# Where the streamed operands of TensorE's matmuls lie in SBUF against their weights

## The reference, cut to what matters

```python
mask = q_bucket[:, :, :, None] == k_bucket[:, :, None, :]
scores = scale * np.matmul(q, k.transpose(0, 1, 3, 2))
scores = np.where(mask, scores, -1000000000.0)
attn = np.exp(scores - max); attn = attn / (sum + 1e-09)
x = attn @ v                                   # (2, 768, 512)
```

```python
x = (sigmoid(causal_conv5(x)) * (x @ w_val)) @ w_out
xk = mu_k * x + (1 - mu_k) * x_prev            # x_prev: the token before
xr = mu_r * x + (1 - mu_r) * x_prev
k = np.maximum(xk @ w_k, 0.0)                  # 512 -> 1024
out = sigmoid(xr @ w_r) * (k * k @ w_v)        # 1024 -> 512
```

## Time and profile before

| | us |
|---|---|
| median of 3 runs | 484.28 (484.23 to 484.29) |
| the profiled execution | 484.03 |
| its span | 482.2 |
| TensorE matmul rows busy | 472.4 (98%) |
| TensorE weight-load rows busy | 401.4 (83%) |
| VectorE, ScalarE, GpSimd busy | 345.7, 279.4, 259.8 |
| TensorE on the chain that ended last | 79% of the span |
| scores L688, 384 matmuls | 92.1 busy, 361 ns each |
| dense matmuls L735 and L743, streamed 256 columns | 277 to 283 ns each |

### The profile page before, as it was taken

One profiled execution on the slowest core, in us unless ns is written; L12 is line 12 of the kernel. 1 busy time (PEld: TensorE's weight loads), 2 busy tenths in 40 slices (PEclk: granted clock), 3 DMA queues, 4 the chain that ended last, 5 costly groups with the idle time before them and its releaser, 6 DMA issues.

```text
span 482.2 us, 9492 instructions
## 1 busy us (share of the span) xinstructions
PE 472.4 (98%) x3541; PEld 401.4 (83%) x3541; DVE 345.7 (72%) x607; ACT 279.4 (58%) x597; POOL 259.8 (54%) x258
## 2 busy tenths in 40 slices
PE   7899999999999999999999999999999999999997
PEld 6766767676676776777779999999999999999997
DVE  5887897988888888887747977876678579326211
ACT  5977878878787987876745541442443353344230
POOL 5795647374472745652197673575455457346140
PEclk9999999999999999999999999999999999999999
DMA  6210310304021030200220001001000000100101
GB/s 231 67 55 18 113 41 5 135 17 137 16 68 72 17 136 18 71 19 18 88 87 1 3 1 44 1 1 46 2 2 32 13 2 1 45 1 2 44 1 44
DMA packets 10557, 20.69 MB, mean 43 GB/s; under 512 B 1680, under 2 KB 6928, under 8 KB 10512
## 3 DMA queue, kind: packets, MB, share of 16 engines
q1 hardware_dynamic: 10224, 19.94, 12.4%
q10 hardware_dynamic: 288, 0.15, 0.1%
HBM read 16.94 MB, written 3.15 MB: 42 GB/s over the span
## 4 chain that ended last, share of the span: by engine, by line
PE 79%; DVE 9%; issue 5%; ACT 3%; POOL 2%; DMA 1%; SPq 0%; DVEq 0%; POOLq 0%; ACTq 0%
PE ps L735 29%; PE ps L723 14%; PE ps L743 12%; PE ps L699 10%; PE ps L688 10%; ACT probs L500 2%; PE ps L709 2%; DVE gate L923 1%; DVE tmp_b L1014 1%; DVE negmax L880 1%; DVE pt L887 1%; PE ps L671 1%; DVE x L913 1%; PE ps L662 1%; DMA raw_k<-kT 1%
## 5 line engine op out<-in xcount | busy, mean ns | idle before, releaser
L880 DVE TENSOR_REDUCE negmax<-ps 128x1 f32<-128x768 f32 x96 | 91.7, 956 | 23.6 <-PE ps L688 22.9
L688 PE MATMUL ps<-k,q 128*128 128x384 f32 x384 | 92.1, 361 | 3.4 <-ACT probs L500 2.8
L500 ACT ACTIVATE probs<-ps,negmax 128x768 f32<-128x768 f32 x96 | 86.6, 902 | 10.2 <-DVE negmax L880 9.9
L699 PE MATMUL ps<-ident,probs 128*128 128x128 f32 x576 | 82.3, 275 | 1.2
L699 PEld LDWEIGHTS ps<-ident,probs 128*128 128x128 f32 x576 | 66.8, 140 | 11.9 <-DVE pt L887 4.7
L688 PEld LDWEIGHTS ps<-k,q 128*128 128x128 f32 x384 | 62.7, 189 | 15.3 <-ACT probs L500 10.6
L723 PE MATMUL ps<-pt,vals 128*64 128x384 f32 x384 | 68.8, 494 | 0.0
L450 POOL TENSOR_TENSOR h_lo<-tmp_b,h_hi 128x256 fp32r<-128x256 f32 x48 | 38.9, 816 | 45.3 <-ACT h_hi L602 45.3
L508 ACT ACTIVATE pt<-ps 128x384 f32<-128x384 f32 x96 | 47.0, 489 | 18.7 <-PE ps L699 15.0
L887 DVE COPY pt<-ps 128x384 f32<-128x384 f32 x96 | 52.1, 542 | 2.8 <-PE ps L699 2.8
L735 PE MATMUL ps<-xk_hi,w_hi 128*128 128x256 f32 x192 | 53.7, 280 | 0.0
(11 more groups left out here) (86 smaller groups left out, 1105.4 us busy)
## 6 DMA issues: line engine op xcount, KB each, us to landing
w_raw<-w SPq DMA_DIRECT2D x8, 640.0 KB, 6.4
raw_q<-qT SPq DMA_DIRECT2D x8, 384.0 KB, 5.2
raw_k<-kT SPq DMA_DIRECT2D x8, 384.0 KB, 3.2
vals<-v SPq DMA_DIRECT2D x16, 192.0 KB, 2.4
out<-w_raw SPq DMA_DIRECT2D x24, 128.0 KB, 1.7
w_raw<-w SPq DMA_DIRECT2D x4, 512.0 KB, 3.3
codes_b<-codes ACTq DMA_DIRECT2D x1, 128.0 KB, 4.2
proj_bd<-proj ACTq DMA_DIRECT2D x1, 16.0 KB, 3.3
```

The source lines that it names most:

```text
L500: act.activation(probs[par][:, :], score[par], ACT.Exp, bias=negmax[:, t:t + 1], accum_out=sums[:, t, 0:1]).then_inc(exp_done, 1)
L688: last = pe.matmul(ps[:, 2 * par + half, 0:HALF], qq[h][:, q], kk[h][:, half * HALF:(half + 1) * HALF], start=first, stop=not first)
L699: last = pe.transpose(tbank[u][:, k * P:(k + 1) * P], probs[g % 2][:, kt * P:(kt + 1) * P], ident[:, :])
L880: dve.tensor_reduce(negmax[:, t:t + 1], score[g % 2], AX.XY, ALU.max, negate=True).then_inc(max_done, 1)
```

## The change

Only declarations change, so only addresses. In the attention a set is declared as `q1`, `q2`, a filler of 64 bytes (`KEYS_BEHIND`), `k1`, `k2`, and after the three sets a filler of 320 bytes rounds the fillers up to 512. In the dense part the filler before `x_hi` becomes 288 bytes, the one before `y_hi` goes, the one before `h_hi` becomes 64, the one before `xk_hi` 448, and the one before `xr_hi` goes. Program order, waits and transfers are as before.

```diff
+KEYS_BEHIND = (64, 64, 64)
...
-        def apart(name, size):
+        def apart(name, size, stack=ctx):
 
-            sb(f"apart_{name}", [P, size // 4])
+            sb(f"apart_{name}", [P, size // 4], F32, stack)
...
             q1[s] = sb(f"q1_{s}", [P, SEQ], F32R, att)
+            q2[s] = sb(f"q2_{s}", [P, SEQ], F32R, att)
+            apart(f"k_{s}", KEYS_BEHIND[s], att)
             k1[s] = sb(f"k1_{s}", [P, SEQ], F32R, att)
-            q2[s] = sb(f"q2_{s}", [P, SEQ], F32R, att)
             k2[s] = sb(f"k2_{s}", [P, SEQ], F32R, att)
+        apart("sets", -sum(KEYS_BEHIND) % 512, att)
...
-        apart("x", 256)
+        apart("x", 288)
         x_hi, x_lo = sb("x_hi", [P, DT, GQ], F32R), sb("x_lo", [P, DT, GQ], F32R)
-        apart("y", 448)
         y_hi, y_lo = sb("y_hi", [P, DT, GQ], F32R), sb("y_lo", [P, DT, GQ], F32R)
...
-        apart("h", 288)
+        apart("h", 64)
         h_hi, h_lo = sb("h_hi", [P, FT, GQ], F32R), sb("h_lo", [P, FT, GQ], F32R)
-        apart("xk", 32)
+        apart("xk", 448)
         xk_hi, xk_lo = sb("xk_hi", [P, DT, GQ], F32R), sb("xk_lo", [P, DT, GQ], F32R)
-        apart("xr", 288)
         xr_hi, xr_lo = sb("xr_hi", [P, DT, GQ], F32R), sb("xr_lo", [P, DT, GQ], F32R)
```

## The result

The changed kernel takes 486.00 us (median of 7 runs, 485.86 to 486.33), the kernel before 484.28 us: 1.0033 times as long, interval 1.0023 to 1.0044. It is slower, by 1.7 us, where 6.0 us less was forecast. Its profiled execution took 485.88 us.

A forecast was written before the change was run, and what follows sets the result against it. The prediction took TensorE's start-to-start matmul time as the bound in the dense part; savings of 4.4 + 0.5 + 1.1 = 6.0 us gave 478.3 us. Its range was 475.0 to 482.3 us.

The forecast's parts named there:

- What bounds the kernel: TensorE's stream of load and matmul pairs in the dense part; layout can move the time from start to start.
- Step A: From 317.2 us on: all x, y, xk and h stages fall to 113.3 ns a matmul, 4.4 us less.
- Step B: From 235 to 317.2 us: 2.2 us by the same arithmetic, mostly lost in waits, so 0.5 us less.
- Step C: Attention scores: 8.3 ns less a matmul with keys 64 behind queries; a third counts, 1.1 us less.
- slow lock: Rival: after the wait at 317.21 us the dense stream stays at 117.9 ns a matmul; 485.8 us, chance 0.09.
- stages near 118 ns: Sign that the forecast is wrong: dense stages at 118 ns a matmul, pointing to the slow lock.
- scores still at 175 ns: Sign that the forecast is wrong: attention score matmuls still start 175 ns apart, instead of 166 to 168.

The follow-up runs named there:

- xk_288: The changed kernel with xk_hi and xk_lo moved back to 288 behind their weights, all else at 64; 482.38 us.
- w0_64: The changed kernel with w2 at the place of w1 modulo 512, dense operands still 64 behind their weights; ten executions from 479.6 to 485.8 us, ratio 0.9988.
- keys_only: The kernel before with only the attention's new sets, dense fillers as before; 483.78 us, ratio 0.9994 (0.9985 to 1.0003).
- kick: The changed kernel, no address changed, with one extra small matmul ahead of the y stage of chunks 2, 3, 4 and 5; 485.77 us.
- w0_192: The changed kernel with w2 at the place of w1 modulo 512 and all dense operands at 192; ten executions from 478.9 to 485.8 us, ratio 0.9968.
- w0_192_kick: w0_192 with one extra matmul of 128 columns ahead of the y stage of chunk 2; median 479.72 us, ratio 0.9936.
- x_32: The changed kernel with x alone at 32 behind its weights; twelve executions, eight of them at 485.6 to 486.1 us, ratio 1.0012.

## Why the prediction was wrong

**What bounds the kernel** held: the distance from one dense matmul's start to the next is the time of the second half, and all of the 1.8 us came from it.

**Step A failed, the forecast -4.4 us, measured +1.8 us.** It took 113.3 ns for a property of the offset 64, because five of six xr stages had it. Those five were no five witnesses: each was entered the same way, from an xk at 288 in its changing rhythm (starts 113 to 120 ns apart, 116.7 on average), in one execution. The sixth, entered from a wait by way of a steady xk, was the other state of the same layout, and the changed kernel's profile has that state in 27 of its 30 dense stages. An xk in the changing rhythm is no guarantee either: in xk_288 the one at 299.93 us was followed by a long xr. The arithmetic behind it was sound: w0_64 shows 1392 matmuls at 113.3 ns in its short executions and a time of 479.6 to 480.0 us.

**Step B** was tested only in part. The y and x from 249 us on were short, and nearly all of their gain went into the wait behind them: x's last start to xk's first grew from 0.25 to 0.65 us, and xk began 0.07 us earlier, where 0.1 us was forecast. The stages from there to 317 us were long, and the wait there shrank instead of growing: y began 0.05 us later, not 0.5 us earlier.

**Step C was mis-sized.** The excess of the scores was to fall by 8.3 ns a matmul. In the changed kernel they are still (105.80 - 105.45) / 2 = 175 ns apart in the tile that the earlier trace rows shows for before, and the attention's 213 us hold the same 1354 matmuls.

```profile
105.45 0.33 PE L689 MATMUL ps<-k,q 128*128 128x384 f32 x1
...
105.63 0.33 PE L689 MATMUL ps<-k,q 128*128 128x384 f32 x1
...
105.80 0.34 PE L689 MATMUL ps<-k,q 128*128 128x384 f32 x1
```

keys_only bounds the effect by its interval to 0.7 us less, where 1.1 us was forecast. The excess taken from streams of 256 columns did not carry over to streams of 384; why, no run shows.

**The rival "slow lock"** named the outcome and its size: 485.8 us, measured 486.0, with +0.88 us for xr, +0.62 for h and +0.46 for xk; from the stage starts they are 4 x 48 x 4.5 = 0.86, 480 x 1.2 = 0.58 and 384 x 1.0 = 0.38 us. That its total fits so well is partly luck: it holds 0.5 us back from the scores, which did not come, and its stages add up to 2.0 us where 1.8 came. It got a chance of 0.09, by counting stages. Its account of where the rhythm is decided was half right. The wait at 317 us can give either rhythm (w0_64 is the same program with either), but in the changed kernel it would hardly matter if the boundary from h to x ends a short one there as it did in xk_288 and kick, at the same addresses. The forecast looked at the offset of each stage and not at the one stream and load that meet across two stages.

Of the signs that the prediction named, stages near 118 ns and scores still at 175 ns came true.

**What stays open.** What makes 64 and 192 good and 0 and 96 bad, what puts a stage after a wait into one rhythm or the other, and whether any entry can force the short one. Only steps of 32 bytes were tried, several in one execution each. No short execution of w0_192, w0_192_kick or x_32 was profiled.

## What to carry to other kernels

A distance between starts seen in one stage may be one of two stable states of the same layout; before a layout is changed for it, look how each stage with that distance was entered, and treat stages that follow each other in one execution as one observation. When streams and weights are laid out against each other, the boundary between two stages counts as well: from h to x the good state lasted only in the kernels with a filler that put both sets of weights at one place, three executions against four. And time such a change in ten or more executions: seven agreed in the changed kernel, while its neighbour w0_64 gave 480 and 486 us from one program.

## What the runs showed of the hardware

- The time of a 256-column matmul with its own load of 128 weights depends on the distance between the streamed tile and the weights, from 113.3 to 120.0 ns at a granted clock of 1.00, with a period of 256 bytes in the offsets seen.
- At 64 and at 192 it has two values, 113.3 and 117.8 ns, at 288 three, 116.7, 117.9 and 120.0 ns. At 64 each held over hundreds of matmuls: 113.3 ns from 317.6 us to the end in w0_64's profile, 117.8 ns from 260.5 us to the end in the changed kernel's.
- One program can take either from execution to execution, 479.6 or 485.8 us in w0_64, at a granted clock of 1.00.
